# Two chunks of the first expert's weights split by ScalarE and VectorE instead of GpSimd, and the zeros of y and two weight loads issued at other places

## Chip, cores, metric

One NeuronCore of a Trainium2 chip runs the whole program. The metric is the device time of one execution in microseconds (us). The profile adds one execution of its own, with its trace.

## What is computed

Three stages follow one another, all in float32:

```
# 1. attention, window 64, B,H,S,D = 4,8,576,64
scores = where(0 <= i-j < 64, q @ k.T / 8, -1e9);  x = softmax(scores) @ v      # x: [2304, 512]
# 2. mixture of experts, top 2 of 8
noisy = x @ w_gate + log1p(exp(x @ w_noise)) * noise
top2, their softmax weights g
for e in range(8):
    for k in range(2):
        rows = top2[:, k] == e
        out[rows] += g[rows, k] * (maximum(x[rows] @ w1[e], 0) @ w2[e])         # w1: 512x1024, w2: 1024x512
# 3. feed-forward
h = out @ w_in;  result = (h * clip(h + 3, 0, 6) / 6) @ w_out                   # 512x2048, 2048x512
```

## The kernel before

**Order.** Attention runs over 18 tiles of 128 tokens (`T` = 0 to 17). The routing is done in five lots of tiles (`LOTS`): tiles 0 to 2, 3 to 6, 7 to 10, 11 to 13 and 14 to 17. For each lot VectorE works out the row of every token in the buffer `x_sorted` in HBM (`route`, parts 0 to 7, the row numbers go to `slot_cur` and raise `slots_ready`), and GpSimd then writes each tile twice by an indirect DMA (`scatter(t, k)`, line 723, semaphore `x_sent`). In `x_sorted` each expert has a region of its own. After the attention come eight experts and then the feed-forward layer.

**An expert.** It takes five blocks of up to 128 tokens (`x_in`), in two parts: part 0 has blocks 0 to 2, part 1 has blocks 3 and 4. TensorE turns a block (`turn_x`, line 1624), ScalarE and VectorE split it into a high and a low half in fp32r (`x_hi` line 907, `x_lo` line 1215). For each part eight steps follow, c = 0 to 7: `hidden(c)` (line 1640) multiplies by w1, ScalarE and VectorE apply the ReLU and split (`h_hi` line 917, `h_lo` line 1221), and `project(c-1)` (line 1657) multiplies by w2 into the Y banks. Each product is three passes over the halves. In expert 0 the blocks 3 and 4 are turned between `project(6)` and `project(7)` of part 0, since their rows can only be read when all lots have been scattered. In part 1 TensorE turns the next expert's blocks 0, 1 and 2 after `hidden` of c = 2, 4 and 6, each time before the `project` of that step.

**Weights.** SyncE (SP) loads a set of eight chunks of 512 KB (0 to 3 are w1, 4 to 7 are w2) through four places of `stage`: chunk c goes to place c mod 4 and waits until chunk c-4 has been split, which the semaphore `w_ready` counts. A chunk is split into `W` by two instructions, a high half (`split_hi`, line 692, counts `w_half`) and a low half (`split_lo`, line 702, counts `w_ready`). Before the change GpSimd does this for all eight experts; for the first expert in four pieces each, chunks 0 to 2 between scatters, and chunks 3 to 7 in one run after the scatters of lot 2, with copies of the last x tiles (`keep_x`, line 733) in between. Only then come the 14 scatters of tiles 11 to 17. `project(4)` of part 0 waits for chunk 6, `project(6)` for chunk 7. ScalarE and VectorE split w_out's first four chunks later in the kernel in the same form (`out_hi` line 964, `out_lo` line 1377).

**SyncE's order around the change.** In the loop over T it loads the first expert's chunks (`load_first`, chunk 7 at T = 17) and writes zeros to y_sorted in 1 MB pieces (`zero_y`, line 528). Then it loads expert 1's chunks 0 to 3 (each waits for `w_ready`), writes the last two pieces of zeros, writes zeros behind expert 0's rows (`pad(0, ...)`, line 588, two blocks), waits for all scatters and for that pad, loads blocks 3 and 4 of `x_in` (line 602), writes zeros behind expert 1's rows (`pad(1, ...)`, five blocks, 1280 KB), and loads expert 1's chunks 4 to 7 (line 572). Every one of these DMAs goes out on SyncE's queue.

**Who waits for pad(1).** In part 1 of expert 0, ScalarE does after `h_hi` of c = 0

```
act.wait_ge(padded[1 - par], ...)      # pad(1) has landed
for j in range(PARTS[1][0]):
    load_x(e + 1, j)                   # x_in of expert 1, line 882
for j in (0, 1): store_y(e, j, base)   # line 929
```

and only then `h_hi` of c = 1.

**Last scatter and GpSimd.** After its last scatter GpSimd waits until all have landed and begins with expert 1's eight chunks (their place in `W` lies over `x_cur`, the source of the scatters).

## Time and profile before

| | us |
|---|---|
| median of 3 runs | 1030.97 |
| lowest, highest | 1029.88, 1043.11 |
| the profiled execution, its own time | 1022.32 |
| its span in the trace | 1020.5 |
| TensorE busy in the span | 987.1 (97%) |
| VectorE, ScalarE, GpSimd busy | 417.2, 228.2, 427.5 |

A time in the rows is counted from the start of the span. Engines: PE is TensorE's matmul stream, DVE is VectorE, ACT is ScalarE, POOL is GpSimd, SPq and ACTq are the DMA issues of SyncE and ScalarE. The profiled execution was quicker than any of the three timed ones, so differences worked out in the trace are set against the median as differences.

### The profile page before, as it was taken

Reading aid. Unit: us, or ns where it says so; the run is one execution under the profiler, and the core shown is the slowest. Engines: PE = TensorE matmul, PEld = TensorE weight load, DVE = VectorE, ACT = ScalarE, POOL = GpSimd, SP = SyncE. Lnnn points to the kernel's source line nnn. Section 1 sums busy time; section 2 is a strip of 40 time slices with the busy share of each in tenths; the row PEclk is TensorE's granted clock in tenths of the full one; section 3 lists DMA queues with packets and bytes.
Section 4 is the critical chain, followed back from the end, with each engine's and each line's share of the span. In section 5 each row is a group of like instructions: output and inputs, shape, how many; then the busy total and the mean of one; then the engine's idle time right before and its main releaser. Section 6 shows DMA issues by size and latency. Waiting matters only on the chain.

```text
span 1020.5 us, 18019 instructions
## 1 busy us (share of the span) xinstructions
PE 987.1 (97%) x7108; PEld 875.2 (86%) x7108; DVE 417.2 (41%) x897; ACT 228.2 (22%) x537; POOL 427.5 (42%) x331
## 2 busy tenths in 40 slices
PE   6999895999999999999999999999999999999998
PEld 5777684889889898999889888999999999999997
DVE  3688671312222221312222246535445445355333
ACT  4766510111111111111111122111111111111111
POOL 4177696994755829193755829200101001000000
PEclk9999997999999999999999999999999999999999
DMA  9789759854362717153342434200101111000000
GB/s 179 163 204 251 236 161 301 254 187 153 109 210 84 210 61 217 68 179 140 111 158 83 137 105 142 63 31 21 42 31 41 32 40 41 31 1 1 32 1 31
DMA packets 124822, 115.94 MB, mean 114 GB/s; under 512 B 63824, under 2 KB 92464, under 8 KB 124752
## 3 DMA queue, kind: packets, MB, share of 16 engines
q1 hardware_dynamic: 104160, 75.06, 26.4%
q10 hardware_dynamic: 14768, 21.01, 6.2%
q0 software_dynamic: 5824, 18.91, 5.6%
q8 instruction: 47, 0.77, 0.3%
q14 instruction: 23, 0.19, 0.1%
HBM read 75.90 MB, written 39.06 MB: 113 GB/s over the span
## 4 chain that ended last, share of the span: by engine, by line
PE 87%; POOL 5%; DVE 3%; DMA 2%; SPq 1%; issue 1%; ACT 0%; DVEq 0%; POOLq 0%; ACTq 0%
PE PS L1657 20%; PE PS L1777 20%; PE PS L1640 19%; PE PS L1761 19%; POOL x_sorted L723 2%; PE PS L1520 2%; PE PS L1624 2%; POOL W L702 1%; POOL W L692 1%; PE PS L1499 1%; SPq L506 1%; PE PS L1435 1%; PE PS L1483 1%; PE PS L1702 1%; DMA k_later<-in_k_dram 1%
## 5 line engine op out<-in xcount | busy, mean ns | idle before, releaser
L1657 PE MATMUL PS<-W,hs_room 128*128 128x512 f32 (+1 forms) x960 | 246.6, 400 | 0.1
L1640 PEld LDWEIGHTS PS<-xs,W 128*128 128x128 f32 x1536 | 229.2, 188 | 10.9 <-issue 0.4
L1640 PE MATMUL PS<-xs,W 128*128 128x256 f32 (+2 forms) x1536 | 238.0, 305 | 0.0
L1777 PE MATMUL PS<-W,gs 128*128 128x512 f32 x864 | 217.0, 395 | 0.9 <-DVE gs L1371 0.9
L1761 PE MATMUL PS<-x2s,W 128*128 128x384 f32 x1152 | 216.6, 337 | 0.0
L1761 PEld LDWEIGHTS PS<-x2s,W 128*128 128x128 f32 x1152 | 201.3, 188 | 7.2
L692 POOL TENSOR_TENSOR W<-stage,ones_f 128x1024 fp32r<-128x1024 f32 (+1 forms) x100 | 147.5, 1485 | 139.4 <-PE PS L1657 134.6
L1657 PEld LDWEIGHTS PS<-W,hs_room 128*128 128x128 f32 (+1 forms) x960 | 173.0, 187 | 35.7 <-DVE hs_room L1221 0.3
L1777 PEld LDWEIGHTS PS<-W,gs 128*128 128x128 f32 x864 | 161.2, 188 | 31.8 <-issue 1.6
L702 POOL TENSOR_TENSOR W<-stage,W 128x1024 fp32r<-128x1024 f32 (+1 forms) x100 | 185.7, 1867 | 5.9
L1221 DVE SCALAR_TENSOR_TENSOR hs_room<-PS,hs_room 128x256 fp32r<-128x256 f32 (+2 forms) x128 | 61.9, 484 | 288.7 <-ACT hs_room L917 288.7
L917 ACT ACTIVATE hs_room<-PS 128x256 fp32r<-128x256 f32 (+2 forms) x128 | 55.3, 432 | 371.0 <-PE PS L1640 354.2
L1030 ACT ACTIVATE gs<-PS 128x384 fp32r<-128x384 f32 x96 | 47.2, 492 | 307.3 <-DVE PS L1369 307.3
L801 POOL DMA_INDIRECT ya<-y_sorted,slot x18 | 18.9, 1050 | 223.6 <-PE PS L1702 199.7
L1367 DVE TENSOR_SCALAR hc<-PS 128x384 f32<-128x384 f32 x96 | 53.5, 557 | 130.9 <-PE PS L1761 130.9
L1371 DVE SCALAR_TENSOR_TENSOR gs<-PS,gs 128x384 fp32r<-128x384 f32 x96 | 53.6, 558 | 60.6 <-ACT gs L1030 60.6
L1369 DVE SCALAR_TENSOR_TENSOR PS<-hc,PS 128x384 f32<-128x384 f32 x96 | 54.0, 562 | 3.3
L723 POOL DMA_INDIRECT x_sorted<-x_cur,slot_cur x36 | 35.4, 983 | 14.7 <-issue 8.5
L848 ACT ACTIVATE probs<-PS,negmax 128x128 f32<-128x128 f32 x144 | 39.4, 400 | 0.0
L1215 DVE TENSOR_TENSOR xs<-PS,xs 128x512 fp32r<-128x512 f32 (+1 forms) x40 | 27.2, 680 | 28.2 <-ACT xs L907 26.7
L1624 PE MATMUL PS<-ident,x_in 128*128 128x128 f32 (+1 forms) x160 | 24.8, 279 | 13.0 <-DMA x_in<-x_sorted 13.0
L1234 DVE COPY y_sb<-PS 128x512 f32<-128x512 f32 (+1 forms) x40 | 27.0, 689 | 22.7 <-PE PS L1657 21.7
(139 smaller groups left out, 560.4 us busy)
## 6 DMA issues: line engine op xcount, KB each, us to landing
stage<-in_moe_w_dram SPq DMA_DIRECT2D x64, 512.0 KB, 3.8
x_sorted<-zeros SPq DMA_DIRECT2D x7, 1280.0 KB, 7.4
y_sorted<-y_sb ACTq DMA_DIRECT2D x33, 256.0 KB, 3.0
x_in<-x_sorted ACTq DMA_DIRECT2D x31, 256.0 KB, 4.1
out_dram<-o_sb SPq DMA_DIRECT2D x18, 256.0 KB, 2.1
vD<-in_v_dram SPq DMA_DIRECT2D x68, 64.0 KB
stage<-in_moe_w_in_dram SPq DMA_DIRECT2D x8, 512.0 KB, 4.0
stage<-in_moe_w_out_dram SPq DMA_DIRECT2D x8, 512.0 KB, 4.4
```

Source lines behind the costliest of these rows:

```text
L692: last = nc.gpsimd.tensor_tensor(chunk_at(parity, c, 0)[:, at], stage[:, c % STAGES, at], ones_f[:].broadcast_to([P, n]), ALU.mult)
L702: last = nc.gpsimd.tensor_tensor(chunk_at(parity, c, 1)[:, at], stage[:, c % STAGES, at], chunk_at(parity, c, 0)[:, at].bitcast(F32), ALU. ...
L723: pool.indirect_dma_start(out=x_sorted, out_offset=bass.IndirectOffsetOnAxis(ap=slot_cur[:, k, t:t + 1], axis=0), in_=x_cur[:, t, :], in_o ...
L917: nc.scalar.activation(hs[:, c % 2, 0, 0:n], HP_[:, c % 2, 0:n], ACT.Relu).then_inc(hhi_done, 1)
L1221: nc.vector.scalar_tensor_tensor(hs[:, c % 2, 1, 0:n], HP_[:, c % 2, 0:n], 0.0, hs[:, c % 2, 0, 0:n].bitcast(F32), ALU.max, ALU.subtract). ...
L1367: nc.vector.tensor_scalar(hc[:, c % 2], h, 3.0, 0.0, ALU.add, ALU.max).then_inc(hc_done, 1)
L1369: nc.vector.scalar_tensor_tensor(G6[:, c % 2], hc[:, c % 2], 6.0, h, ALU.min, ALU.mult).then_inc(g6_done, 1)
L1371: nc.vector.scalar_tensor_tensor(gs[:, c % 2, 1], G6[:, c % 2], 1.0 / 6.0, gs[:, c % 2, 0].bitcast(F32), ALU.mult, ALU.subtract).then_inc( ...
L1640: last = nc.tensor.matmul(HP_[:, c % 2, 0:n], W[:, par, 0, b, at:at + P], xs[part][:, a, kd, 0:n], start=start, stop=(kd == KD - 1 and (a, ...
L1657: last = nc.tensor.matmul(Y[0:n, first + t, :], hs[:, c % 2, a, t * P:t * P + n], W[:, par, 1, b, c * DM:(c + 1) * DM], start=(c == 0 and ...
L1761: last = nc.tensor.matmul(H2P[:, c % 2, :], W[:, 0, kd // 2, b, at:at + P], x2s[par][:, a, kd, :], start=first, stop=(kd == KD - 1 and (a, ...
L1777: last = nc.tensor.matmul(OP[:, tt, :], gs[:, c % 2, a, tt * P:(tt + 1) * P], W[:, 1, c // FC, b, at:at + DM], start=(c == 0 and (a, b) == ...
```

## The change

GpSimd no longer splits chunks 6 and 7 of the first expert (`BESIDE = 2`). ScalarE makes their high halves after its `h_hi` of c = 2 and c = 3 in expert 0, part 0 (`beside_hi`), and VectorE makes both low halves after `h_lo` of c = 4 (`beside_lo`); its `tables()` and `places_in_y()` move one step later, to c = 5 and c = 6. GpSimd raises `w_half` by two in their place, so that its later waits count right. All four pieces of zeros for y are written in the loop over T (one at 16, three at 17, after the load of chunk 7), and expert 1's chunks 2 and 3 are loaded after the loads of `x_in` and before `pad(1, ...)`, for they need the places of `stage` that chunks 6 and 7 hold.

```diff
+    BESIDE = 2
-    ZERO_AT = (16, 17)
+    ZERO_AT = (16, 17, 17, 17)
...
-                if T in ZERO_AT:
-                    zero_y(ZERO_AT.index(T))
+                for n in range(ZERO_PARTS):
+                    if ZERO_AT[n] == T:
+                        zero_y(n)
...
-            load_expert(1, 0, QCH)
-            for n in range(len(ZERO_AT), ZERO_PARTS):
-                zero_y(n)
+            load_expert(1, 0, QCH - BESIDE)
             sp.wait_ge(pads_ready, 1)
             pad(0, 0, 0, PARTS[1][1])
             wait_sent(sp, 0, NB - 1)
             sp.wait_ge(padded[0], 16 + 1)
             for j in range(PARTS[1][0], BLOCKS):
                 sp.dma_start(x_in[:, j], x_sorted[block_row(0, j):block_row(0, j) + P, :]).then_inc(x_loaded[j], 16)
+            load_expert(1, QCH - BESIDE, QCH)
             pad(1, 1, 0)
             load_expert(1, QCH)
...
-            for c in range(len(SPLIT_AT), SCH):
+            for c in range(len(SPLIT_AT), SCH - BESIDE):
                 first_there(c)
                 split_hi(0, c, PIECES)
                 split_lo(0, c, c + 1, PIECES)
-                if kept < TILES:
-                    keep_x(kept)
-                    kept += 1
+                keep_x(kept)
+                kept += 1
             assert kept == TILES
+            pool.sem_inc(w_half, BESIDE)
...
+            def beside_hi(c):
+                act.wait_ge(stage_full[c % STAGES], 16 * (c // STAGES + 1))
+                at = slice((c - QCH) * CH, (c - QCH + 1) * CH)
+                nc.scalar.copy(W[:, 0, 1, 0, at], stage[:, c % STAGES, :]).then_inc(beside_half, 1)
...
+                    if first and c in (2, 3):
+                        beside_hi(SCH - BESIDE + c - 2)
...
+            def beside_lo(c):
+                at = slice((c - QCH) * CH, (c - QCH + 1) * CH)
+                dve.wait_ge(w_ready, c)
+                dve.wait_ge(beside_half, c - (SCH - BESIDE) + 1)
+                nc.vector.tensor_tensor(W[:, 0, 1, 1, at], stage[:, c % STAGES, :], W[:, 0, 1, 0, at].bitcast(F32),
+                                        ALU.subtract).then_inc(w_ready, 1)
...
                     if first and c == 4:
+                        for n in range(SCH - BESIDE, SCH):
+                            beside_lo(n)
+                    if first and c == 5:
                         tables()
                         dve.wait_ge(tabs_ready, 1)
-                    if first and c == 5:
+                    if first and c == 6:
                         places_in_y()
                         route(NB - 1, 7)
```

## Rows read from the trace of the kernel before

**Rows 1.** Timeline of PE: start, length, line, operation, idle before.

```profile
150.65 2.25 PE L1657 MATMUL PS<-W,hs_room 128*128 128x512 f32 x9
...
158.84 2.25 PE L1657 MATMUL PS<-W,hs_room 128*128 128x512 f32 x9
173.34 1.12 PE L1624 MATMUL PS<-ident,x_in 128*128 128x128 f32 x4 [12.24 <-DMA x_in<-x_sorted]
174.72 1.12 PE L1624 MATMUL PS<-ident,x_in 128*128 128x128 f32 x4 [0.26 <-DMA x_in<-x_sorted]
175.49 3.69 PE L1657 MATMUL PS<-W,hs_room 128*128 128x512 f32 x9
179.01 2.99 PE L1640 MATMUL PS<-xs,W 128*128 128x256 f32 x24
...
184.66 0.60 PE L1624 MATMUL PS<-ident,x_in 128*128 128x128 f32 x4
185.28 1.66 PE L1657 MATMUL PS<-W,hs_room 128*128 128x512 f32 x6
```

**Rows 2.** Timeline of POOL, 85 to 171 us.

```profile
119.11 0.97 POOL L723 DMA_INDIRECT x_sorted<-x_cur,slot_cur  x1 [0.30 <-issue]
...
137.29 0.62 POOL L733 COPY x_cur<-x_new 128x512 f32<-128x512 f32 x1
...
148.47 1.02 POOL L723 DMA_INDIRECT x_sorted<-x_cur,slot_cur  x1 [0.15 <-issue]
...
165.12 0.97 POOL L723 DMA_INDIRECT x_sorted<-x_cur,slot_cur  x1 [0.30 <-issue]
170.86 1.89 POOL L692 TENSOR_TENSOR W<-stage,ones_f 128x1024 fp32r<-128x1024 f32 x1 [4.77 <-DMA x_sorted<-x_cur,slot_cur]
```

**Rows 3.** Timeline of ACT, 118 to 205 us.

```profile
122.43 1.33 ACTq L882 DMA_DIRECT2D x_in<-x_sorted  x3
...
180.69 1.32 ACTq L882 DMA_DIRECT2D x_in<-x_sorted  x3
...
184.38 0.39 ACT L917 ACTIVATE hs_room<-PS 128x256 fp32r<-128x256 f32 x1 [3.37 <-issue]
```

**Rows 4.** Timeline of DVE, 118 to 205 us.

```profile
145.37 0.16 DVE L1172 CAST slot_cur<-slot_f 128x8 int32<-128x8 f32 x1
147.34 0.54 DVE L1221 SCALAR_TENSOR_TENSOR hs_room<-PS,hs_room 128x368 fp32r<-128x368 f32 x1 [1.81 <-ACT hs_room L917]
...
151.43 0.54 DVE L1221 SCALAR_TENSOR_TENSOR hs_room<-PS,hs_room 128x368 fp32r<-128x368 f32 x1 [0.53 <-ACT hs_room L917]
...
152.54 0.42 DVE L1297 TENSOR_TENSOR moved<-moved,blk 128x252 f32<-128x252 f32 x1
```

**Rows 5.** Operations on stage: shortest/median/longest ns, first and last start.

```profile
L964 ACT CAST W<-stage x4: 1037/1046/1052, 608.2 to 615.3; 128x1024 fp32r<-128x1024 f32 x4
L1377 DVE TENSOR_TENSOR W<-stage,W x4: 1215/1220/1259, 609.2 to 619.5; 128x1024 fp32r<-128x1024 f32 x4
```

**Rows 6.** One-us windows: busy us of each engine, PE clock, DMA share, GB/s.

```profile
116.00:117.00 1.00, 0.24 (x2) 0.14 (x2) 0.86 (x8) 0.92 (x3) 0.69 (x2) 1.00 1.05 311
117.00:118.00 1.00, 0.94 (x5) 0.97 (x6) 0.15 (x1) 0.00 (x0) 0.70 (x2) 0.52 1.03 363
122.00:123.00 1.00, 0.92 (x61) 0.95 (x64) 0.93 (x9) 0.09 (x1) 0.98 (x2) 1.00 0.03 8
164.00:165.00 1.00, 0.00 (x0) 0.00 (x0) 0.00 (x0) 0.00 (x0) 0.81 (x1) 0.91 1.07 354
```

**Rows 7.** Timeline of SP's DMA issues, 120 to 200 us.

```profile
148.72 4.32 SPq L528 DMA_DIRECT2D y_sorted<-zeros  x2
...
172.25 0.57 SPq L588 DMA_DIRECT2D x_sorted<-zeros  x1
```

**Rows 8.** DMA issues between 172.2 and 172.4 us: KB, us to landing.

```profile
x_sorted<-zeros SPq DMA_DIRECT2D x1, 1280.0 KB, 7.3
```

**Rows 9.** Tile y_sorted, 148.7 to 149.5 us: landing of its two writes.

```profile
DMA to landing us min/median/max: 8.8/12.0/15.2
```

More of the change, by code:

```diff
@@ L330, in attention_moe_ffn @@
         w_ready = sem("w_ready")
+        beside_half = sem("beside_half")
         x_loaded = [sem(f"x_loaded{j}") for j in range(BLOCKS)]
```

## The prediction

> **What bounds the kernel now.** I read the page's busy shares first (they stand in the table above): TensorE is busy 97% of the span, so time is to be had only where it stands still or runs at the lower clock, and its timeline says where. One pause stands out, 12.24 us ahead of the turn of block 3 at 173.34 us [rows 1]. Before it `project(6)` ends at 158.84 + 2.25 = 161.09. The pause is put down to the DMA into `x_in`, so I followed that back: SyncE loads blocks 3 and 4 when all scatters have landed, and GpSimd starts those 14 scatters at 148.47 and the last at 165.12, one every 1.28 us [rows 2]. Ahead of them stand chunks 3 to 7. So this stage is set by GpSimd's queue and by what lies behind the last scatter. I count from the moment S at which GpSimd sees the scatters landed and begins its next split, 170.86 [rows 2], 5.74 us after the start of the last scatter.
>
> **The pause also costs clock.** In the 12 us the granted clock falls from 2.4 to 1.2 GHz (0.91 of full speed over 164 to 165 us, when TensorE had stood still since 161.1) [rows 6]. `project(7)` then takes 3.69 us where `project(6)` took 2.25, and a turn 1.12 where the one at 184.66 took 0.60 [rows 1]: 1.44 + 0.52 = 1.96 us lost after the pause.
>
> **GpSimd's part of the change.** It drops four groups, chunks 6 and 7. The last copy of x that must come before is at 137.29 for 0.62 us; with 0.15 us to the first scatter these begin at 138.06, not 148.47: 10.41 us earlier [rows 2]. Six of them are of tiles whose places have long been there; they end at 138.06 + 6 x 1.28 = 145.7. The other eight need lot 4's `slots_ready`, written at 145.37 + 0.16 = 145.53 [rows 4], 0.2 us ahead; this is the next thing that would hold GpSimd. The last scatter starts at 154.71.
>
> **Landing of the last scatter.** Between two rows: 5.74 us as now, when 2 MB of zeros for y and a pad went out in the same stretch (the issue of two pieces begins at 148.72 [rows 7]), and 3.32 us, from the last scatter of lot 2 at 119.11 [rows 2] to the loads that wait for it at 122.43 [rows 3], where the DMA engines were 3% busy between 122 and 123 [rows 6]. The zeros now go out near 126 us, and of the pads only the small one is near. I take 4.1, nearer to the empty case since only scatters are left: S = 158.8, 12.1 us earlier.
>
> **The splits beside.** ScalarE needs 1.05 us for a high half, VectorE 1.22 for a low one [rows 5]. ScalarE does them after `h_hi` of c = 2 and 3; the steps are 4.1 us apart (147.34 to 151.43 for `h_lo` [rows 4]) and its own part of one is about half a us, so there is room, at no cost. VectorE begins at the end of `h_lo(4)`, 147.34 + 0.46 = 147.8 (its next operation begins there): low half 6 is done at 149.1, low half 7 at 150.4. `project(4)`, which needs chunk 6, starts at 150.65 [rows 1]: 1.5 us to spare. `h_lo(5)` comes at 151.43 [rows 4], so VectorE is free again. `tables()` now stands in that place; between `h_lo(4)` and the end of its idle time at 151.43 - 0.53 it took 3.1 us, and the steps leave 4.1 - 0.5 us, so both moved blocks fit. Cost nil, covered by TensorE's `hidden` and `project`; if the cover went, each us past 150.65 would cost one.
>
> **A rule that speaks against this.** During VectorE's 0.42 us with two inputs in SBUF at 152.54 [rows 4] the scatters kept their step of 1.28 us [rows 2]. The Trainium skill, "SBUF — State Buffer", in its part on engine ports, states that a VectorE instruction with two SBUF inputs and a GpSimd one that reads SBUF shut each other out for whole instructions. By that rule the two low halves could hold the scatters by up to twice 1.22 us, and the gain below would be 2.4 us smaller; the row shows nothing of the kind, and I take nil.
>
> **SyncE's queue.** The last two pieces of zeros move from 148.7 to about 127. Ahead of them is chunk 7's load, which ScalarE wants only after `h_hi` of c = 3; behind them chunks 0 and 1 of expert 1, wanted after S, and the pad of expert 0, which can go when VectorE has written `pad_row`, before the 145.37 of rows 4, and has until S. The issue itself blocks SyncE, 4.32 us for two [rows 7], with nothing due. Cost nil.
>
> **What is late next.** Turn of block 3 at S + 2.48 = 161.3, so the pause of 12.24 us shrinks to about 0.2. Block 4 is turned 1.38 us later, and `hidden(0)` of part 1, at 179.01 = S + 8.15 before [rows 1], comes at S + 8.15 - 1.96 = 165.0 if the clock stays. Up to here the gain is 12.1 + 1.96 = 14.0 us. The edit that takes some of it back is the pair of loads placed ahead of `pad(1)`. That pad was issued at 172.25 = S + 1.39 [rows 7] and landed 7.3 us later [rows 8], at S + 8.7; ScalarE came for it with its loads of the next `x_in` at 180.69 = S + 9.8 [rows 3], so there was 1.1 us of slack. Now ScalarE comes at S + 9.8 - 1.96 = S + 7.9, and the pad goes out behind two loads of 512 KB. These cost at least their issue, 0.8 us, and at most 6.9 us, the distance at which the second of two 1 MB writes of zeros landed behind the first (15.2 + 0.54 - 8.8 [rows 9]). At the 354 GB/s of a full stretch [rows 6] 1 MB takes 3.0 us; I take this, since the queue was drained in order in rows 9 and these loads have longer runs than the zeros. The pad lands at S + 11.7 = 170.5, and ScalarE waits 3.8 us. Queued behind this wait on ScalarE are the x loads, two stores of y and `h_hi(1)`; for these TensorE waits in its turn of expert 1's block 0 and in `project(1)`. From loads to `project(1)` it took 185.28 - 180.69 = 4.59 us, so `project(1)` starts at 170.5 + 4.6 = 175.1 instead of 185.28: 10.2 us gained, 3.8 of the 14.0 given back.
>
> **Clock in the new pause.** TensorE would stand idle for about 3.8 us around 171 to 175, in two pieces. It was full speed until 117 us, when after 0.24 us of work in the us before it fell to 0.52 [rows 6]; so it may fall here. Price between nothing and the 1.96 of above. Since part of the low stretch lies in the pause, I take 0.8. Sum: 10.2 - 0.8 = 9.4 us.
>
> **From there on** TensorE is the chain to the end, and every later wait is on something that has moved with it. Span 1020.5 - 9.4 = 1011.1; profiled execution 1022.32 - 9.4 = 1012.9; median 1030.97 - 9.4 = 1021.6.
>
> **The rivals.**
> - *The pad is hidden.* The two loads drain beside it and it lands at S + 9.5: 1.6 us of wait and no fall of the clock. Gain 14.0 - 1.6 = 12.4, time 1018.6. For it: SyncE issues a load in under 0.4 us. Against: the order in rows 9. 0.16.
> - *The scatters don't profit fully.* The three pieces of zeros reach into the stretch from 138 us, or the places of lot 4 or the low halves hold GpSimd, so that S comes 2 to 4 us later than reckoned, and the clock falls with full price: 9.4 - 3 - 1.2 = 5.2, time 1025.8. For it: 5.74 us at present and the margin of 0.2 us. This also stands for a change that doesn't take its full effect. 0.17.
> - *Slower, by the pad alone.* If `pad(1)`, 1280 KB in short runs behind 1 MB, goes at the pace of the second piece of zeros, 15.2 us for 1 MB [rows 9], it lands 19 us after its issue at S + 2.2 = 161.0, at 180. Then the loads of `x_in` start where they did before, the pause has only moved from the middle of the expert to its second part, and two falls of the clock come on top: 0.6 gained, 2.0 lost, time 1032.4. It decides from a landing at about 178.7. Against: rows 9 had the scatters beside them, the pad has none. 0.05.
> - My forecast has the rest, 0.62, with its own range from 1018 to 1026 (landing 3.3 to 5.7, loads 0.8 to 6.9, clock 0 to 1.96).
>
> **Range and chances.** 1016.5 to 1030: from the hidden pad with an early landing to most of the second rival; the three runs before lie up to 12 us above the lowest, which widens both ends by about 2. A measurement of this kernel tells about 2%, 20.6 us, from no change. No case reaches it on the quick side, even 14.0 + 0.8 falls short; on the slow side none either. So within 2%: 0.97, faster 0.02, slower 0.01.
>
> **What would show it.** First scatter of tile 11 near 138.1, last near 154.7; GpSimd's next split at 158.1 to 160.5; TensorE's pause before the turn of block 3 under 2 us and full clock after it; low halves done before 150.65. Then, for the forecast, a new wait of 2 to 5 us on `x_in` before the turn of expert 1's block 0, with ScalarE idle until `pad(1)` lands some 11.7 us after S. Without that wait the rival of the hidden pad is right. The prediction is wrong if VectorE's blocks collide with `h_lo`, if the pad lands past 175, or if something later in the kernel takes the time back.

## The result, and the profile after

| | before | after |
|---|---|---|
| median of 14 runs each, us | 1030.72 | 1035.69 |
| lowest, highest | 1026.52, 1047.47 | 1033.37, 1038.66 |
| profiled execution, its time and span | 1022.32, 1020.5 | 1038.66, 1036.7 |

The ratio after to before is 1.0055, 95% interval 1.0037 to 1.0072: 5.0 us slower at the medians, where 9.4 us quicker was forecast. It is outside the range of 1016.5 to 1030, though within the 2% that had been given 0.97.

The profiles are each one execution, and these two are not alike: before's is quicker than all of its 14 timed runs, after's is the slowest of its 14, so that their spans lie 16.2 us apart and the medians 5.0. Timeline of PE, after (start, length, line, operation, idle before):

```profile
118.76 0.74 PE L1520 MATMUL PS<-ident,probs 128*128 128x128 f32 x4
126.60 1.09 PE L1553 MATMUL PS<-ident,x_new 128*128 128x128 f32 x4 [7.10 <-issue]
...
146.17 1.11 PE L1645 MATMUL PS<-ident,x_in 128*128 128x128 f32 x4 [4.26 <-DMA x_in<-x_sorted]
...
151.27 4.03 PE L1661 MATMUL PS<-xs,W 128*128 128x368 f32 x12
...
182.84 2.25 PE L1678 MATMUL PS<-W,hs_room 128*128 128x512 f32 x9
185.25 1.29 PE L1645 MATMUL PS<-ident,x_in 128*128 128x128 f32 x8 [0.15 <-DMA x_in<-x_sorted]
...
188.47 2.99 PE L1661 MATMUL PS<-xs,W 128*128 128x256 f32 x24
...
198.63 1.11 PE L1645 MATMUL PS<-ident,x_in 128*128 128x128 f32 x4 [4.36 <-DMA x_in<-x_sorted]
```

The pause before the turn of block 3, 12.24 us in [rows 1], is gone (0.15 us at 185.25), as forecast. But `project(6)`, at 182.84, is 24.0 us later than before (158.84), and even the turn of block 3, with no pause ahead of it, is 11.9 us later. The cause lies before the first expert: TensorE stands 7.10 us still between tiles 16 and 17, put down to "issue", which no row of the profile before has. The expert then waits 4.26 us for `x_in`, and once more 4.36 us in part 1. VectorE stands in the same place, released by "remote". Timeline of DVE, after:

```profile
125.68 0.69 DVE L1096 TENSOR_REDUCE negmax<-PS 128x4 f32<-128x512 f32 x1 [7.18 <-remote]
```

Two windows of after for the pause and the ten us behind it (length, then busy us of PE, its weight loads, DVE, ACT and POOL, granted clock of PE, DMA share, GB/s):

```profile
119.00:125.00 6.00, 0.50 (x4) 0.26 (x3) 0.00 (x0) 0.00 (x0) 4.63 (x6) 0.69 1.02 315
127.00:137.00 10.00, 7.92 (x154) 6.11 (x152) 7.59 (x17) 5.23 (x15) 9.84 (x17) 0.67 0.32 109
```

TensorE works 0.50 us in six, VectorE and ScalarE not at all, and behind the pause the mean clock is 0.67 of full speed.

Timelines of SP's and ACT's issues, and the list of DMA issues (KB, us to landing) for the `x_in` loads, after:

```profile
133.53 7.45 SPq L531 DMA_DIRECT2D y_sorted<-zeros  x3
...
183.02 0.90 SPq L576 DMA_DIRECT2D stage<-in_moe_w_dram  x2
184.69 0.57 SPq L592 DMA_DIRECT2D x_sorted<-zeros  x1
```

```profile
138.43 1.60 ACTq L885 DMA_DIRECT2D x_in<-x_sorted  x2
```

```profile
x_in<-x_sorted ACTq DMA_DIRECT2D x2, 256.0 KB, 8.0
```

Three pieces of zeros, 3 MB, go out at 133.53, and `x_in` of part 0 is asked for at 138.43, behind them: it lands 8.0 us later. In the profile before, the issue was at 122.43 [rows 3]. Timeline of POOL, after:

```profile
144.38 0.61 POOL L736 COPY x_cur<-x_new 128x512 f32<-128x512 f32 x1
152.91 1.02 POOL L726 DMA_INDIRECT x_sorted<-x_cur,slot_cur  x1 [7.92 <-DVE slot_cur L1182]
...
169.30 0.97 POOL L726 DMA_INDIRECT x_sorted<-x_cur,slot_cur  x1 [8.97 <-DVE slot_cur L1182]
...
171.85 2.01 POOL L726 DMA_INDIRECT x_sorted<-x_cur,slot_cur  x1 [0.31 <-issue]
...
179.27 0.97 POOL L726 DMA_INDIRECT x_sorted<-x_cur,slot_cur  x1 [0.30 <-issue]
182.36 1.89 POOL L695 TENSOR_TENSOR W<-stage,ones_f 128x1024 fp32r<-128x1024 f32 x1 [2.11 <-DMA x_sorted<-x_cur,slot_cur]
```

GpSimd ends its copies at 144.38 and would be free to scatter, but waits 7.92 us for the slots of lot 3 and 8.97 us for those of lot 4, since VectorE's routing is late as well; the prediction had counted 0.2 us to spare. Then one scatter takes 2.01 us instead of 0.97 (171.85). In the chain of waits of after, the pad is the next thing:

```profile
184.69 9.54 DMA x_sorted<-zeros
...
194.25 4.34 DMA x_in<-x_sorted
```

`pad(1)` landed 9.54 us after its issue behind the two loads (7.3 before [rows 8]).

### The profile page after: what moved, and what is told of

The parts are those of the page before. It is cut to its first block, busy times and chain, and to the rows that moved or that the text cites. A ratio compares the mean times of both kernels' runs of the same rounds, so it can differ in the third digit from the quotient of the medians.

```text
span 1036.7 us, 18010 instructions
## 1 busy us (share of the span) xinstructions
PE 993.6 (96%) x7108; PEld 879.3 (85%) x7108; DVE 417.1 (40%) x899; ACT 230.7 (22%) x539; POOL 417.3 (40%) x315
## 4 chain that ended last, share of the span: by engine, by line
PE 84%; POOL 4%; DMA 3%; issue 3%; DVE 2%; SPq 2%; ACT 0%; another core or an unknown queue 0%; DVEq 0%; POOLq 0%; ACTq 0%
PE PS L1798 19%; PE PS L1678 19%; PE PS L1782 19%; PE PS L1661 18%; POOL x_sorted L726 2%; PE PS L1541 2%; PE PS L1645 2%; SPq L509 1%; PE PS L1504 1%; DMA k_later<-in_k_dram 1%; PE PS L1520 1%; PE PS L1456 1%; DMA x_sorted<-zeros 1%; POOL W L705 1%; PE PS L1723 1%
## 5 line engine op out<-in xcount | busy, mean ns | idle before, releaser
L695 POOL TENSOR_TENSOR W<-stage,ones_f 128x1024 fp32r<-128x1024 f32 (+1 forms) x92 | 142.9, 1561 | 141.2 <-PE PS L1678 138.7
L705 POOL TENSOR_TENSOR W<-stage,W 128x1024 fp32r<-128x1024 f32 (+1 forms) x92 | 179.8, 1963 | 5.8
L1225 DVE TENSOR_TENSOR xs<-PS,xs 128x512 fp32r<-128x512 f32 (+1 forms) x40 | 27.1, 680 | 19.4 <-ACT xs L910 17.8
```

Of the source, the lines that this page charges most:

```text
L695: last = nc.gpsimd.tensor_tensor(chunk_at(parity, c, 0)[:, at], stage[:, c % STAGES, at], ones_f[:].broadcast_to([P, n]), ALU.mult)
L705: last = nc.gpsimd.tensor_tensor(chunk_at(parity, c, 1)[:, at], stage[:, c % STAGES, at], chunk_at(parity, c, 0)[:, at].bitcast(F32), ALU. ...
```

## The experiments

There turned out to be two kinds of executions, told apart by when `x_in` of part 0 is issued. In the **early start** it is at 122 to 126 us (the profile before has 122.43); in the **late start** at 135 to 139 us, with a pause of 5 to 8.4 us at tiles 16 and 17. It went with a whole set of runs: the profile before was an early one, after's a late one. The runs came in five sets; sets 1 and 2 were late in all their profiles, sets 3 to 5 early (sets 1 and 3 were on the same chip). Each ratio is against runs of the kernel before in the same set. The runs of before had medians 1028.17, 1028.84, 1023.23, 1022.85 and 1022.67 us in the five sets. Of the timed runs of before and after themselves there is no trace; that they were late is argued from their medians, which lie 8 and 17 to 19 us above those of the early sets, and from the granted clock averaged over a run of after: 0.985 at the median of the 14, as in the forced late runs of e14 below, where the early ones of e16 have 0.993.

The pause is not the whole of a late start. GpSimd's first scatter of lot 2 waits for VectorE's slots, and it starts before the pause. Timeline of POOL, before, then after:

```profile
109.69 0.97 POOL L723 DMA_INDIRECT x_sorted<-x_cur,slot_cur  x1 [6.17 <-DVE slot_cur L1172]
```

```profile
116.85 0.97 POOL L726 DMA_INDIRECT x_sorted<-x_cur,slot_cur  x1 [9.28 <-DVE slot_cur L1182]
```

This scatter starts at 109.1 to 112.6 us in the early profiles and at 113.1 to 116.9 in the late ones: the attention is already some 3 to 7 us behind the profile before when tile 16 comes, and the pause comes on top.

Times in the table are read from the PE, ACT and POOL timelines of each profile: issue of `x_in` of part 0, first `hidden` of expert 0, turn of block 3, `hidden(0)` of part 1, first step of expert 1. From there to the end it is 816.5 to 818 us in all of them, so what a kernel gains or loses in its profile is decided by that column. "Forced" is a late start made on purpose in an early set, explained below.

| kernel | x_in | hidden(0) | turn 3 | hidden(0), part 1 | expert 1 | span |
|---|---|---|---|---|---|---|
| before, early | 122.4 | 128.9 | 173.3 | 179.0 | 203.1 | 1020.5 |
| e1_before_again, late | 136.0 | 146.0 | 179.9 | 182.9 | 207.7 | 1025.0 |
| after, late | 138.4 | 151.3 | 185.3 | 188.5 | 218.9 | 1036.7 |
| e3_zeros_back, late | 137.3 | 146.8 | 180.2 | 183.4 | 212.9 | 1030.3 |
| e5_beside_alone, late | 135.0 | 141.9 | 174.4 | 177.6 | 203.1 | 1019.7 |
| e15_before_third, early | 122.7 | 129.7 | 173.8 | 179.4 | 204.4 | 1021.7 |
| e16_after_third, early | 122.5 | 130.5 | 163.6 | 166.7 | 198.9 | 1016.3 |
| e13_before_late, forced | 132.6 | 140.0 | 175.6 | 181.2 | 205.5 | 1022.9 |
| e14_after_late, forced | 132.3 | 143.3 | 176.3 | 179.6 | 211.4 | 1028.9 |
| e10_beside_zeros_after_x, early | 123.7 | 130.9 | 165.9 | 170.7 | 194.8 | 1011.5 |

**First set, late start: before again, and the change in parts.** `e1_before_again` is the kernel before, a single run with its profile.

> The kernel before, unchanged, profiled a second time, because its first profile (span 1020.5 us) was shorter than all its timed runs. Theory A (the three pieces of zeros at T = 17 collide with the first x_in loads): part 0 of expert 0 begins as early against the end of the attention as in the first profile, the first x_in loads land about 3 us after their issue, and the pause before the turn of block 3 is 10 to 13 us; whatever the span has more than 1020.5 lies in the attention, before 130 us. Theory B (the attention merely varies, the change does nothing to it): attention and first hidden step begin up to 15 us later than in the first profile, near the 151 us of the changed kernel.

Measured 1026.78, span 1025.0: the attention and the first hidden step are late in the kernel before too, as theory B had it. Timelines of PE and POOL, e1_before_again:

```profile
122.84 1.09 PE L1532 MATMUL PS<-ident,x_new 128*128 128x128 f32 x4 [5.15 <-issue]
...
177.83 2.25 PE L1657 MATMUL PS<-W,hs_room 128*128 128x512 f32 x9
179.92 1.03 PE L1624 MATMUL PS<-ident,x_in 128*128 128x128 f32 x8
```

```profile
164.73 0.97 POOL L723 DMA_INDIRECT x_sorted<-x_cur,slot_cur  x1 [4.06 <-DVE slot_cur L1172]
...
176.77 1.89 POOL L692 TENSOR_TENSOR W<-stage,ones_f 128x1024 fp32r<-128x1024 f32 x1 [2.12 <-DMA x_sorted<-x_cur,slot_cur]
```

The kernel before has the pause at tile 17 too (5.15 us), so the change doesn't make it. And here TensorE comes to block 3 without any pause: `project(6)` ends at 177.83 + 2.25 = 180.08, while the scatters are seen landed at 176.77. GpSimd itself waits 4.06 us for lot 4's slots. So in this late start nothing of the 12.24 us is there to be gained.

`e2_zeros_alone` is before with the zeros at the new places:

```diff
-    ZERO_AT = (16, 17)
+    ZERO_AT = (16, 17, 17, 17)
```

> The kernel before with the zeros of y alone moved (all four pieces in the loop, at T = 16, 17, 17, 17); splits and weight loads as before. Theory A: the first x_in loads stand behind 3 MB of zeros and take 7 to 8 us instead of 3, part 0 starts 4 to 10 us later, and of that only the shorter landing of the last scatter comes back: slower than before by 3 to 10 us. Theory B: no slower than before, or up to 2 us quicker since the scatters have the DMA engines to themselves. Theory C (the loss is in the loads ahead of pad(1)): same as theory B, since this kernel keeps them in their old place.

Measured 1028.30, 0.9997 (0.9982 to 1.0012): the zeros alone cost the kernel before nothing that can be measured in a late start; theory A had 3 to 10 us.

`e3_zeros_back` is after with the last two pieces back behind expert 1's first loads:

```diff
-    ZERO_AT = (16, 17, 17, 17)
+    ZERO_AT = (16, 17)
...
             load_expert(1, 0, QCH - BESIDE)
+            for n in range(len(ZERO_AT), ZERO_PARTS):
+                zero_y(n)
```

> The changed kernel with the last two pieces of zeros back in their old place, after the loads of the second expert's first chunks; splits beside and the loads ahead of pad(1) as in the changed kernel. Theory A: the first x_in loads take 3 us again, the pause in part 0 stays short, and the kernel is 4 to 9 us quicker than before, 9 to 14 quicker than the changed one. Theory B and theory C: no quicker than the changed kernel, still 3 to 6 us slower than before.

Measured 1030.81, 1.0023 (1.0009 to 1.0037). Of after's 5.0 us, 2.6 remain: not the gain of theory A, and less than the 3 to 6 us of B and C. In the profiles, `x_in` to `hidden(0)` shrinks from 12.8 to 9.6 us.

`e4_pad_first` is after with the pad ahead of the two loads:

```diff
-            load_expert(1, QCH - BESIDE, QCH)
             pad(1, 1, 0)
+            load_expert(1, QCH - BESIDE, QCH)
```

> The changed kernel with pad(1) issued ahead of the two loads of the second expert's chunks 2 and 3, all else as changed. Theory C (these loads in front of the pad are what the change costs): the wait of 4.4 us before the turn of the second expert's block 0 goes, TensorE keeps its clock there, 5 to 6 us quicker than the changed kernel, about as before. Theory A: the wait goes too, but the late start of part 0 stays: 4 to 6 us quicker than the changed kernel, first x_in loads still 7 to 8 us to land. The two theories differ here only in the start of part 0; the time tells what the loads ahead of the pad are worth.

Measured 1030.89, 1.0027 (1.0008 to 1.0045). `hidden(0)` of part 1 to expert 1 took 27.9 us where after took 30.5 and e1 24.8: somewhat less than half the loss of this stretch is gone, while theory C had all of it gone and the time about as before. Of the 3.0 us left, 1.4 are the clock (`project(1)` to expert 1 19.2 us for 17.8 in e1). The rest fits loads that now run beside expert 1's `x_in`, whose first two land 6.0 us after their issue, for 4.3 in e1. Timeline of PE, e4_pad_first:

```profile
191.38 0.91 PE L1645 MATMUL PS<-ident,x_in 128*128 128x128 f32 x4 [2.28 <-DMA x_in<-x_sorted]
```

**Second set, late start: the splits without their side costs.** `e5_beside_alone` is e3 with chunks 2 and 3 of expert 1 loaded ahead of the wait for the scatters:

```diff
             pad(0, 0, 0, PARTS[1][1])
+            load_expert(1, QCH - BESIDE, QCH)
             wait_sent(sp, 0, NB - 1)
...
-            load_expert(1, QCH - BESIDE, QCH)
             pad(1, 1, 0)
```

> The splits beside alone: the changed kernel with the zeros in their old places and the loads of the second expert's chunks 2 and 3 ahead of the wait for all scatters, so that pad(1) has nothing new in front of it. Theory D (in most executions GpSimd does not set part 0: it waits for the places of lot 4, and the x_in loads come just as TensorE ends part 0, as in the second profile of the kernel before): GpSimd now waits some 8 us for lot 4's places, the last scatter is no earlier, time as before within 1.5 us. Theory E (GpSimd's queue sets part 0, as I forecast, and only pad and zeros took the gain away): 5 to 10 us quicker than before.

Measured 1024.01, 0.9956 (0.9935 to 0.9977), 4.8 us quicker than before in the same set: more than theory D allowed (within 1.5 us) and just under theory E (5 to 10). GpSimd does wait in its profile, 7.1 us for lot 4's slots, as D had it. By the ratios of after and e5, 1.0055 and 0.9956, which are of different sets, SyncE's two moves cost some 10 us in a late start; what is left of the change is a gain.

`e6_loads_early` is after with only that move of the loads; `e8_both_mended` is e5 with the first piece of zeros at T = 17 (`ZERO_AT = (17, 17)`, the others as in e5); `e7_first_zero_later` is before with the same `ZERO_AT = (17, 17)`.

> The changed kernel with one edit: the two loads of the second expert's chunks 2 and 3 stand ahead of the wait for all scatters instead of behind the x_in loads. If what remained after putting the pad first was their contention with the x_in loads of the second expert, the turn of that expert's block 0 comes 5.7 us after part 1's first hidden step, as before (10.2 in the changed kernel, 8.1 with the pad first), and the time is 5 to 6 us below the changed kernel's, within 2 us of before. If the contention is not the cause, it stays at 8 and the time is that of the kernel with the pad first, 2.7 us above before.

Measured 1030.53, 1.0016 (1.0001 to 1.0032). With the move of the loads alone the wait for the pad is gone: the turn of expert 1's block 0 comes 5.9 us after `hidden(0)` of part 1, as expected (10.2 in after).

> The kernel before with one edit: the first piece of zeros of y goes out at T = 17 instead of T = 16. Theory F (the pause of 5 to 7 us in tiles 16 and 17, in which TensorE, VectorE and ScalarE all stand, is an instruction fetch that waits behind this piece of zeros and the scatters): the pause goes or shrinks below 2 us, TensorE keeps its clock, part 0 starts 5 to 12 us earlier, and since GpSimd then sets the stage again a pause of up to 12 us appears before the turn of block 3, as in the first profile of before: 0 to 5 us quicker. Theory G (the pause has nothing to do with the zeros): it stays at 5 us or more and the time is as before.

Measured 1028.05, 0.9990 (0.9974 to 1.0006). Timeline of PE, e7_first_zero_later, where no zeros were under way before tile 17:

```profile
124.35 1.09 PE L1533 MATMUL PS<-ident,x_new 128*128 128x128 f32 x4 [6.97 <-issue]
```

The pause is there and as long, 6.97 us, which is theory G. Zeros do not make it.

> Splits beside with both mendings: the first piece of zeros at T = 17, the last two in their old place, the two loads ahead of the wait for all scatters. Theories E or F: the early start of part 0 now meets a GpSimd that is free 10 us sooner, so this is the quickest, 8 to 14 us below before. Theories D and G: as before within 2 us.

Measured 1030.20, 1.0022 (1.0004 to 1.0039). The quickest of all was expected if theories E or F held; it is 1.4 us slower than before, as D and G had it. Read together, e6 and e8, with two or three pieces of zeros just ahead of part 0's `x_in`, are 6 us slower than e5; in the kernel before the same moves cost nothing that can be measured (e2, e7 against before). In the profiles of e2 and e7 `hidden(0)` comes 2.5 and 1.8 us later than in e1, and expert 1 1.7 and 0.6 us later; these are single executions, on two chips. Nor do the profiles show that the zeros are what sets e5 apart: from `x_in` to `hidden(0)` it took 6.9 us, while e1 and e3, with the zeros at the same places as e5, took 10.0 and 9.6, close to the 11.0 of e8. What the zeros cost in a natural late start, 6 us or next to nothing, is not settled.

**Third set, early start.** It was meant to bring the zeros out of both stretches. `e9_before_zeros_after_x` (before) and `e10_beside_zeros_after_x` (e5) write one piece at T = 16 and the other three when `x_in` of part 0 has landed:

```diff
+    ZERO_AT = (16,)
...
             for j in range(PARTS[0][1]):
                 sp.wait_ge(x_loaded[j], 16)
+            for n in range(len(ZERO_AT), ZERO_PARTS):
+                zero_y(n)
             load_expert(1, 0, QCH)
-            for n in range(len(ZERO_AT), ZERO_PARTS):
-                zero_y(n)
```

> The kernel before with the zeros of y from the second piece on issued only when the first three x_in loads have landed. Theory H (zeros ahead of these loads on the queue delay the start of part 0): from the issue of the loads to the first hidden step 6.5 to 8 us instead of 10 and more; as part 0 then starts earlier, GpSimd's last scatter binds and a pause of 2 to 8 us stands before the turn of block 3: 0 to 3 us quicker than before. Rival (the zeros don't matter there, only the run): still 9 to 12 us to the first hidden step, time as before.

Measured 1020.76, 0.9967 (0.9955 to 0.9979), 2.5 us quicker. S came 3.1 us after the last scatter instead of 5.7; but from the issue of `x_in` to `hidden(0)` it took 9.0 us where the profile before has 6.5 and 6.5 to 8 were expected, so part of the gain was lost again. The pause before block 3 is 6.31 us.

> The splits beside, loads ahead of the wait for all scatters, and the zeros from the second piece on only after the first x_in loads have landed. Theory H with D and E joined (relieving GpSimd pays just when part 0 starts early): early start as in the run above but no pause before block 3, quickest of all, 5 to 9 us below before and 1 to 3 below the kernel with the splits beside alone. Rival: as the splits beside alone, 4 to 5 us below before.

Measured 1013.11, 0.9896 (0.9880 to 0.9912), 10.1 us quicker than before. Timeline of PE, e10_beside_zeros_after_x:

```profile
165.85 1.34 PE L1646 MATMUL PS<-ident,x_in 128*128 128x128 f32 x8 [2.62 <-DMA x_in<-x_sorted]
...
176.35 0.66 PE L1646 MATMUL PS<-ident,x_in 128*128 128x128 f32 x4
```

2.62 us of the pause are left, where none was expected, and the wait in part 1 is gone: part 1 to expert 1 takes 24.1 us. The rest of the pause is a price that the move of the loads seems to have: with the two loads ahead of the wait, the last scatter took 3.7 to 6.7 us from its start to S (e5, e6, e8, e17, e18; 6.7 here), with them behind it 3.1 (after, e3, e4, e12, e14, e16). Only in e11, whose scatters come long after the loads, is it 3.1 with the loads ahead.

`e11_beside_gpsimd_filled` is e5 with 17 idle copies on GpSimd (11.45 us) in the place of chunks 6 and 7, so that only the scatters' start is put back:

```diff
             pool.sem_inc(w_half, BESIDE)
+            for _ in range(17):
+                pause()
```

> The kernel with the splits beside alone, but with 17 copies of an unused tile on GpSimd in the place of chunks 6 and 7 (17 x 0.62 = 10.5 us, what their splitting took). Nothing else differs, so the difference to the splits beside alone is what freeing GpSimd is worth. Theory E (GpSimd's queue sets part 0): 5 to 10 us slower than the splits beside alone. Theory D (GpSimd only waits longer for lot 4's places): same time, still 4 to 5 us quicker than before. Joined (it pays where part 0 starts early): 3 to 5 us slower than the splits beside alone, about as before.

Measured 1022.06, 0.9990 (0.9979 to 1.0000), about as before, as the joined theory had it. Timeline of PE, e11_beside_gpsimd_filled:

```profile
175.48 1.12 PE L1648 MATMUL PS<-ident,x_in 128*128 128x128 f32 x4 [7.38 <-DMA x_in<-x_sorted]
```

A pause of 7.38 us is back, and no gain is left: in an early start it is GpSimd's free time that is worth something, not the splits' place as such. e5 itself wasn't run in an early start, so e11 stands beside after (e12) and e10 of the same set, and e11 wasn't run in a late one, so this does not say where e5's late gain comes from.

`e12_after_again` is after unchanged.

> The changed kernel once more, with its profile. If the segments of its first profile are typical: 27 us from tile 14's gate product to the issue of the x_in loads, 11 to 13 us from there to the first hidden step, no pause before block 3, and 29 to 31 us from part 1's first hidden step to the next expert, of which 4 to 6 us are the wait for pad(1). Time 5 to 6 us above before.

Measured 1017.06, 0.9934 (0.9915 to 0.9954): the very kernel that lost 5.0 us is 6.2 us quicker than before here, where 5 to 6 us slower was expected. This made the start the suspect.

**Fourth set, early start: the start forced late.** `e13_before_late` and `e14_after_late` are before and after with 22 idle writes on VectorE at tile 16 (8.40 us in the DVE timeline of e13); nothing else is changed in either kernel:

```diff
             for T in range(TILES):
+                if T == TILES - 2:
+                    for _ in range(DRAGS):      # 22
+                        step(nc.vector.memset(moved[:], 0.0))
```

> The kernel before with VectorE held up at tile 16 by 22 fills of a tile that it doesn't need yet (about 0.25 to 0.3 us each, 5.5 to 7 us), where most profiles so far show TensorE, VectorE and ScalarE standing for 5 to 7 us. Theory J (whether part 0 starts early or late decides whether GpSimd binds): in executions that would have started early it takes the place of the pause before block 3, so the kernel is slower than before by less than the delay, 1 to 5 us; in executions that have the natural pause anyway it adds its whole length and more, 6 to 10 us. Rival (the pause before block 3 has nothing to do with the start): slower by the delay in either case.

> The changed kernel with the same delay on VectorE at tile 16. Theory J: with the late start GpSimd's freedom is worth nothing and only the wait for pad(1) and the zeros ahead of the first x_in loads are left of the change, so this is 3 to 7 us slower than the delayed kernel before, although the changed kernel without delay may be 6 us quicker than before in the same executions. Rival (the sign of the change follows something else than the start of part 0): against the delayed kernel before it stands as the changed kernel stands against before, without delay.

> The kernel before, a third profile, to see which of the two starts these executions have. Theory J: if it has no pause at tile 16 (x_in loads issued near 122 us) it has 8 to 13 us before the turn of block 3; if it has one (issued near 135), none there.

> The changed kernel, undelayed, on the same chip as the three others. Theory J: if the profile of before beside it has no pause at tile 16, 5 to 8 us quicker than before; if it has one, 4 to 7 us slower. Rival (the sign belongs to nothing in the trace): any mixture of the two.

Measured: e13 1024.35, 1.0012 (1.0000 to 1.0024); e14 1030.80, 1.0073 (1.0060 to 1.0087); e15, a single run of before, 1023.53; e16, after unchanged, 1018.35, 0.9945 (0.9926 to 0.9963). So in one set, on one chip, the change is worth -4.5 us as it is, and +6.45 us when both kernels start part 0 some 10 us later; theory J had 5 to 8 us quicker and 3 to 7 us slower. The forced start is not the natural one in everything: the attention is not behind at lot 2 (first scatter at 110.1 us), and before itself loses only 1.5 us by it, where the late sets lie 5 to 6 us above the early ones. Timelines of PE, first e15_before_third, then e16_after_third:

```profile
160.37 2.25 PE L1657 MATMUL PS<-W,hs_room 128*128 128x512 f32 x9
173.76 2.08 PE L1624 MATMUL PS<-ident,x_in 128*128 128x128 f32 x8 [11.14 <-DMA x_in<-x_sorted]
...
179.38 2.99 PE L1640 MATMUL PS<-xs,W 128*128 128x256 f32 x24
```

```profile
161.47 2.25 PE L1678 MATMUL PS<-W,hs_room 128*128 128x512 f32 x9
163.56 1.22 PE L1645 MATMUL PS<-ident,x_in 128*128 128x128 f32 x8
...
166.71 2.99 PE L1661 MATMUL PS<-xs,W 128*128 128x256 f32 x24
...
177.01 0.66 PE L1645 MATMUL PS<-ident,x_in 128*128 128x128 f32 x4 [4.50 <-DMA x_in<-x_sorted]
178.35 2.93 PE L1678 MATMUL PS<-W,hs_room 128*128 128x512 f32 x6 [0.68 <-DVE hs_room L1231]
```

Pause of 11.14 us against none, `hidden(0)` of part 1 at 179.38 against 166.71, then 4.50 us of wait for the pad. The same with the late start, e13_before_late, then e14_after_late:

```profile
175.60 1.97 PE L1628 MATMUL PS<-ident,x_in 128*128 128x128 f32 x8 [3.60 <-DMA x_in<-x_sorted]
...
181.20 3.18 PE L1644 MATMUL PS<-xs,W 128*128 128x256 f32 x24
```

```profile
138.15 1.11 PE L1649 MATMUL PS<-ident,x_in 128*128 128x128 f32 x4 [1.55 <-DMA x_in<-x_sorted]
...
176.33 1.31 PE L1649 MATMUL PS<-ident,x_in 128*128 128x128 f32 x8
...
189.46 0.66 PE L1649 MATMUL PS<-ident,x_in 128*128 128x128 f32 x4 [4.09 <-DMA x_in<-x_sorted]
190.75 2.93 PE L1682 MATMUL PS<-W,hs_room 128*128 128x512 f32 x6 [0.64 <-DVE hs_room L1235]
```

Here before has only 3.60 us of pause to lose; after starts part 0 later, waits as long for the pad, and ends 5.9 us behind. Issues on SP and ACT, e16_after_third and then e14_after_late (two views each):

```profile
125.75 7.78 SPq L531 DMA_DIRECT2D y_sorted<-zeros  x3
```

```profile
122.54 1.32 ACTq L885 DMA_DIRECT2D x_in<-x_sorted  x3
```

```profile
126.78 8.33 SPq L532 DMA_DIRECT2D y_sorted<-zeros  x3
```

```profile
132.27 2.46 ACTq L886 DMA_DIRECT2D x_in<-x_sorted  x2
```

This is where the zeros stand in the two starts: in the early start the `x_in` loads go out at 122.54, 3.2 us ahead of the three pieces; in the late start SyncE issues the pieces at nearly the same time (126.78), but `x_in` only at 132.27, behind them. From its issue to the first turn it took 5.9 us in e14 and 3.7 in e13.

**Fifth set, early start: does the better kernel hold when late?** `e17_best_late` is e10 with the same 22 writes, `e18_best_again` is e10.

> The splits beside with the two loads ahead of the wait for all scatters and the zeros after the first x_in loads, with the 22 fills on VectorE at tile 16 (8.4 us). Theory K (these two mendings take away what the change costs where part 0 starts late): although delayed it is 1 to 4 us quicker than before without a delay, 2 to 6 below what the delayed kernel before had against before (1.5 us slower), and 8 or more below the delayed changed kernel (8 us slower). Rival (the mendings only help with an early start): 1 to 3 us slower than before, like the delayed kernel before.

> The same kernel without the delay, once more. Early start: 8 to 11 us below before, as in its first timing. If the executions have the pause at tile 16, theory K gives 4 to 8 us below before, at least as much as the splits beside alone had there (4.8).

Measured: e17 1021.26, 0.9982 (0.9970 to 0.9994), 3 us below e13 and 9.5 below e14, which are of the set before; e18 1012.96, 0.9903 (0.9888 to 0.9919). Both are as theory K expected. The version holds at the early start and at the forced late one; in a natural late start it wasn't run.

## Why the prediction was wrong, point by point

**The step that failed** is the one that carries the sum to the median: "median 1030.97 - 9.4 = 1021.6". All terms were worked out in an execution of 1022.32 us and set against runs of 1030. That the profile was quicker than every timed run stood in the table and was passed over as a constant; it was a sign that the timed runs were of another kind, in which the pause of 12.24 us is small or doesn't exist. In e1 TensorE finds block 3 there, in e13 it waits 3.60 us for it; of the gain of 14.0 us up to `hidden(0)` of part 1, e13 to e14 has 1.6, while the costs behind it are 7.5 us. So the change comes out 5.9 us slower there, at the start of expert 1. Had I asked what the 8 us between profile and median could be, a rival "the timed runs start part 0 later" would have been on the list: pause gone, pad and zeros left, slower.

How far each term held is seen in e15 to e16 (early) and e13 to e14 (late):

| term | forecast | early | late |
|---|---|---|---|
| first scatter of lot 3 | -10.4 | -11.2 | -4.7 |
| wait for lot 4's slots | 0 | 3.1 | 8.3 |
| last scatter to S | 4.1 | 3.1 | 3.1 |
| S | -12.1 | -10.2 | +0.8 |
| hidden(0) of part 1 | -14.0 | -12.7 | -1.6 |
| turn of expert 1's block 0, counted from there | +3.8 | +3.5 | +3.9 |
| wait before project(1) | 0 | +0.9 | +0.8 |
| project(1) to expert 1 (clock) | +0.8 | +2.7 | +2.8 |
| start of expert 1 | -9.4 | -5.6 | +5.9 |

In the early start too the sum was 3.8 us too good: 1.3 by `hidden(0)` of part 1, 0.9 by the wait before `project(1)`, put at nothing, and 1.9 by the clock, less 0.3 at the turn.

- **GpSimd's part** held in the early start. The margin of 0.2 us to lot 4's slots was no margin; e16's POOL timeline:

```profile
136.62 0.63 POOL L736 COPY x_cur<-x_new 128x512 f32<-128x512 f32 x1
137.40 1.02 POOL L726 DMA_INDIRECT x_sorted<-x_cur,slot_cur  x1
...
147.92 0.97 POOL L726 DMA_INDIRECT x_sorted<-x_cur,slot_cur  x1 [3.13 <-DVE slot_cur L1182]
...
160.95 1.90 POOL L695 TENSOR_TENSOR W<-stage,ones_f 128x1024 fp32r<-128x1024 f32 x1 [2.11 <-DMA x_sorted<-x_cur,slot_cur]
```

  They begin 11.2 us earlier, and 3.13 us of it are spent waiting at 147.92. From the first of the 14 to the last it takes 20.48 us (137.40 to 157.88) against 16.75 in e15 (148.62 to 165.37), 3.7 more: this wait of 3.1, less the usual 0.3 between two scatters, and 1.0 for the long scatter beside the low halves. The last one lands 2.7 us quicker: -11.2 + 3.7 - 2.7 = -10.2.
- **Landing** with the zeros gone was 3.1 us, quicker than the 4.1 that I took, and by 0.2 us than the 3.32 of the empty case: with only scatters left, the empty row was the one to follow. The zeros needn't be gone for it: e1, with two pieces issued at 153.50 and the last scatter at 173.67, has 3.1 as well.
- **The splits beside** cost nothing, as forecast. In e16 the low halves end at 150.42 + 2.48 = 152.90 and `project(4)` starts at 153.28; in after 174.27 and 174.65. That is the second of the two; chunk 6, which `project(4)` waits for, is done half of those 2.48 us earlier, so its margin was 1.6 us for the 1.5 reckoned.
- **The pad** was sized right, 3.5 to 3.9 us for 3.8, at both starts (4.6 in e16 against the first profile of before, since e15 itself is 1.2 us longer there). It landed 11.9 us after S in after and 12.8 in e16, for 11.7. With the loads moved ahead of the wait (e5, e6, e10) its extra is gone.
- **The clock** after that pause was under-sized, 2.7 us for 0.8, above the upper end of 1.96 that I gave. It came only where the wait for the pad was: `project(1)` to expert 1 is 17.8 us in all profiles without that wait, 19.2 to 19.5 in after, e3 and e4, and 20.5 to 20.6 in e12, e14 and e16.
- **SyncE's queue, "Cost nil"**, was wrong in one of the two cases. I named chunk 7's load ahead of the zeros and the loads behind them on SyncE, but not ScalarE's `x_in` loads, which go out on another queue and share the DMA engines. Early they are ahead of the three pieces; late they are behind: 2.2 us to the turn, 3.2 us to `hidden(0)` (140.0 in e13, 143.3 in e14), part of it clock, for a turn took 1.11 us in e14 and 0.60 in e13.
- **The rivals.** "The scatters don't profit fully" was nearest in the early start (5.2 reckoned, 4.5 and 6.2 measured), and its signs were there: the slots of lot 4 and the low halves held GpSimd, and the clock fell with more than full price. The slower rival had the right place, the pad, but not the mechanism: no pad of 19 us, but a gain that was not there.
- Nothing later takes time back: expert 1 to the end is 816.5 to 818 us in every profile.

**What stays open.** Why part 0 starts early in some sets of runs and late in others: not by the zeros (e7), not by the change (e1), not by the chip alone (one late and one early set on one chip). Since the attention is behind before tile 16, the cause is not to be sought in the pause alone. Of the 9.8 us by which e5's expert 1 starts before e3's, 4.0 lie in the pad's stretch, which the move of the loads explains; 2.3 are an earlier `x_in` and 2.6 its shorter way to `hidden(0)`, perhaps a difference between sets, and the rest lies up to part 1. So why e5 beats before even in a late start, when e1 has no pause for it to remove, is not shown. After itself wasn't timed in the set of e3 and e4, and before's own median was 2.6 us lower there (1028.17 for 1030.72), so the sizes of e3 and e4 against after carry the difference between two sets of runs. And no natural late start has before and after in one set beyond the first measurement.

## What to carry to other kernels

When the profiled execution is quicker or slower than all timed runs, find out what differs before a gain is counted in it: a pause that you mean to remove may not exist in the runs that are timed. Try a change at both ends of a start that varies, by delaying one engine on purpose; e13 and e14 turned an argument about chance into one pair of numbers. And of a transfer moved in a queue ask which loads of any other queue are then behind it, in each of the orders that can occur: zeros placed after the loads have landed, with the loads of weights moved as well (e10, e17), gained at the early start and at the forced late one.

## What the runs showed of the hardware

- **A pause of three engines.** In natural late starts TensorE, VectorE and ScalarE stand still together at tiles 16 and 17, TensorE for 5.15 us (e1, e3) to 8.43 us (e6), with "issue" or "remote" as releaser in most of them. The granted clock behind it is 0.67 of full speed over ten us in after, and 0.50, which is the level of 1.2 GHz, in e1 over 123 to 133 us. The DMA engines were all busy in the pause of after (share 1.02), but in e7 only 0.56 over 118 to 124 us, with the same pause. No run shows what the engines waited for.
- **Two inputs in SBUF.** I had taken nil for the low halves' effect on the scatters. Timeline of DVE, after:

```profile
171.80 2.47 DVE L1239 TENSOR_TENSOR W<-stage,W 128x1024 fp32r<-128x1024 f32 x2
```

  The scatter that starts at 171.85, 0.05 us after the first of the two, takes 2.01 us instead of 0.97 (POOL timeline above), 1.04 us more, the better part of one low half's 1.22. The same stands in every other kernel with `beside_lo` but e10 (1.96 to 2.02 us), and in none without it, where the longest scatter took 1.10 us (e15). In e10 a scatter began 0.02 us after the first low half and took 0.96, and the two low halves took 2.55 us instead of 2.47. The held scatter is as the Trainium skill, "SBUF — State Buffer", in its part on engine ports, describes it, an instruction of one engine held for one of the other. The prediction's estimate by that page was up to 2.4 us; the traces show 1.0, once in each of those executions. The row that I had relied on was of an instruction of 0.42 us at 152.54, inside a scatter that took 1.00 us instead of 0.97. Timeline of POOL, before:

```profile
152.35 1.00 POOL L723 DMA_INDIRECT x_sorted<-x_cur,slot_cur  x1 [0.30 <-issue]
```

  So an overlap that short, 0.2 us into a scatter, says nothing about one of 1.22 us that starts just before it.
- **Zeros and small loads.** 256 KB of `x_in` took 3.0 us to land in the profile before, where they went out ahead of the zeros, and 8.0 us in after, behind 3 MB of zeros whose issue another queue had begun 4.9 us before. Behind one piece they took 3.5 us (e13, issued 5.8 us before) and 5.0 (e1, 4.7 us before), behind three 6.0 (e14, 5.5 us before).
